# Scores: six of 24 chunks as products of parts, squares in PSUM, norms per partition

## The reference

```python
qn = q / (np.linalg.norm(q, axis=1, keepdims=True) + 1e-06)
kn = k / (np.linalg.norm(k, axis=1, keepdims=True) + 1e-06)
s = kn.transpose(0, 2, 1) @ qn / tau
s = s - s.max(-1, keepdims=True)
a = np.exp(s)
a /= a.sum(-1, keepdims=True) + 1e-09
return (v @ a)
```

## Time and profile before

| | |
|---|---|
| median of 3 runs | 999.54 us (999.44 to 999.87) |
| profiled execution | 1000.11 us, its span 998.3 us |
| PE busy | 992.4 us, 99% |
| DVE, ACT, POOL busy | 852.2, 763.8, 60.4 us |
| granted TensorE clock | 1.00 |
| chain that ended last | PE 97%, DMA 1% |

### The profile page before, as it was taken

One profiled execution on the slowest core, in us unless ns is written; L12 is line 12 of the kernel. 1 busy time (PEld: TensorE's weight loads), 2 busy tenths in 40 slices (PEclk: granted clock), 3 DMA queues, 4 the chain that ended last, 5 costly groups with the idle time before them and its releaser, 6 DMA issues.

```text
span 998.3 us, 14814 instructions
## 1 busy us (share of the span) xinstructions
PE 992.4 (99%) x5355; PEld 899.4 (90%) x5355; DVE 852.2 (85%) x1051; ACT 763.8 (77%) x1181; POOL 60.4 (6%) x55
## 2 busy tenths in 40 slices
PE   9999999999999999999999999999999999999998
PEld 8888989999999999999999888888888888888997
DVE  7779989999999999999896777887888888888886
ACT  6689888999999989999886676666666666666664
POOL 0200001101001011010110000000000000000000
PEclk9999999999999999999999999999999999999999
DMA  9913233635527436353445632543534434434333
GB/s 348 377 23 74 43 59 43 123 95 79 113 40 133 110 51 123 91 78 102 76 52 179 154 112 74 153 105 122 151 79 151 116 95 139 140 95 132 112 98 92
DMA packets 154116, 113.15 MB, mean 113 GB/s; under 512 B 114880, under 2 KB 137536, under 8 KB 154048
## 3 DMA queue, kind: packets, MB, share of 16 engines
q1 hardware_dynamic: 140704, 96.26, 32.6%
q0 software_dynamic: 12736, 15.50, 11.8%
q10 hardware_dynamic: 608, 0.49, 0.2%
HBM read 77.07 MB, written 35.16 MB: 112 GB/s over the span
## 4 chain that ended last, share of the span: by engine, by line
PE 97%; DMA 1%; issue 0%; SPq 0%; DVE 0%; ACT 0%; POOL 0%; DVEq 0%; POOLq 0%
PE banks L1371 50%; PE banks L1572 21%; PE banks L1510 15%; PE banks L1484 7%; PE banks L1381 2%; DMA early_w_in<-w_in 1%; PE banks L1607 0%; PE banks L1399 0%; PE banks L1481 0%; PE banks L1615 0%; SPq L521 0%; SPq L524 0%; ACT early_w_in_parts L427 0%; PE banks L1414 0%; DVE out_tile L1361 0%
## 5 line engine op out<-in xcount | busy, mean ns | idle before, releaser
L1371 PE MATMUL banks<-x_parts,w_in_parts 128*128 128x512 f32 (+1 forms) x1152 | 274.9, 375 | 0.0
L1371 PE MATMUL banks<-xT_parts,a_w_in 128*128 128x512 f32 (+1 forms) x1152 | 259.4, 375 | 0.1
L1371 PEld LDWEIGHTS banks<-x_parts,w_in_parts 128*128 128x128 f32 x1152 | 215.6, 189 | 28.4 <-issue 0.7
L1572 PE MATMUL banks<-g_pair_parts,w_forms 128*128 128x512 f32 (+1 forms) x987 | 239.3, 375 | 0.0
L1371 PEld LDWEIGHTS banks<-xT_parts,a_w_in 128*128 128x128 f32 x1152 | 212.8, 189 | 23.5 <-issue 0.5
L914 ACT ACTIVATE g_pair<-banks 128x512 f32<-128x512 f32 (+1 forms) x192 | 113.0, 588 | 125.2 <-PE banks L1371 118.2
L1572 PEld LDWEIGHTS banks<-g_pair_parts,w_forms 128*128 128x128 f32 x987 | 186.5, 189 | 22.1
L1258 DVE TENSOR_TENSOR g_pair_parts<-g_forms,g_pair_parts 128x1024 fp32r<-128x1024 f32 (+1 forms) x96 | 115.2, 1201 | 23.3 <-ACT g_pair_parts L923 23.1
L1083 DVE SCALAR_TENSOR_TENSOR g_raw<-g_raw,banks 128x1024 f32<-128x1024 f32 (+1 forms) x96 | 114.9, 1197 | 21.0 <-ACT g_raw L792 20.3
L923 ACT ACTIVATE g_pair_parts<-g_forms 128x1024 fp32r<-128x1024 f32 (+1 forms) x96 | 99.4, 1036 | 33.9 <-PE banks L1572 33.3
L792 ACT ACTIVATE g_raw<-g_raw 128x512 f32<-128x512 f32 (+1 forms) x192 | 119.5, 622 | 5.9
(11 more groups left out here) (117 smaller groups left out, 981.8 us busy)
## 6 DMA issues: line engine op xcount, KB each, us to landing
w_forms<-w_forms SPq DMA_DIRECT2D x48, 896.0 KB, 4.7
w_forms<-w_out_forms SPq DMA_DIRECT2D x8, 896.0 KB, 4.2
early_qk<-q SPq DMA_DIRECT2D x23, 256.0 KB, 7.4
early_qk<-k SPq DMA_DIRECT2D x22, 256.0 KB, 7.8
y_raw<-y_parts SPq DMA_DIRECT2D x10, 512.0 KB, 5.4
x_parts<-y_raw SPq DMA_DIRECT2D x40, 128.0 KB, 4.8
out<-out_tile SPq DMA_DIRECT2D x40, 128.0 KB, 2.7
v_in<-v SPq DMA_DIRECT2D x36, 128.0 KB, 4.1
```

What stands on the lines that cost most here:

```text
L1371: mm = pe.matmul(dst, lhsT, rhs, start=first and n == 0, stop=last and n == len(todo) - 1)
L1572: mm = pe.matmul(m_banks[m][:, 0:u.n], ring[k % N_RING][:, form, x, :], by_turns(gp2[k % 2][:, y, operand, 0:u.n]), start=k == 0 and part ...
```

## The change

Six chunks (2, 5, 8, 11, 14, 17) are turned into parts by GpSimd (a copy to `float32r`, then a subtraction) and multiplied by `product`, 12 products in place of 4. Four buffers `early_qk_parts` hold them. PE takes the split chunks in pairs and later than the others: 0, 1, 3, 4, 6, 7, then 2 and 5, and so on. A chunk load into the buffer of a split chunk waits for the split instead of the product. All chunk products read Q from two halves in turn, so the score columns lie in another order, which DVE turns back as it scales them.

ACT writes the squares to PSUM, three pairs of banks (`NSQ` = 3), and DVE adds from there. The sum of one row of the sums to the other is gone: the norm products (`norm_sums`) add both rows in PSUM. These give all sums of q and k with one value to a partition, four columns in bank 2, eight products of one column. One root, one reciprocal of four columns. To have the norms of q along a row again, DVE multiplies the identity by them (two diagonals of 128x128), PE multiplies these by ones (`rq_rows`, bank 7), and DVE copies the result to SBUF. The norm products stand one chunk later than before, `rq_rows` behind the first chunk of head 1. GpSimd starts on w_in1 without waiting for the norms; ACT's roundings of pieces 1 to 3 stand further back.

The second piece of w_in1 moved behind the table load, the third behind the first transposed block, the fourth behind the second exponential. The diff, cut to its core:

```diff
-NQ, NSQ = 14, 4
+NQ, NSQ = 14, 3
+SPLIT = (2, 5, 8, 11, 14, 17)
+N_PARTS = 4
...
+        squares = lambda c: two_banks[1 + c % NSQ][:, :, 0:CHUNKS[c] * C].rearrange("p x (r c) -> p x r c", c=C)
+        turn_of = lambda c: SPLIT[SPLIT.index(c) // 2 * 2 + 1] + 2.5 if c in SPLIT else c
+        IN_BOTH = sorted(range(BOTH), key=turn_of)
+        multiplied = lambda c: IN_BOTH.index(c) + 1
+        def free_parts(eng, c):
+            n = SPLIT.index(c)
+            if n >= N_PARTS:
+                eng.wait_ge(c_mm, multiplied(SPLIT[n - N_PARTS]))
+        part_chunk = lambda c, part: qk_parts[SPLIT.index(c) % N_PARTS][:, part, :, 0:CHUNKS[c], :]
...
-                    sp.wait_ge(c_mm, c - NQ + 1)
+                    if c - NQ in SPLIT:
+                        sp.wait_ge(c_lo, SPLIT.index(c - NQ) + 1)
+                    else:
+                        sp.wait_ge(c_mm, multiplied(c - NQ))
...
-            pool.wait_ge(x_dve, at_dve["q_eps"])
+            for n, c in enumerate(SPLIT):
+                for x in (Q, K):
+                    pool.wait_ge(d_qk[c % NQ][x], qk_loaded(c))
+                free_parts(pool, c)
+                pool.tensor_copy(part_chunk(c, 0), raw_chunk(c)).then_inc(c_hi, 1)
+                pool.wait_ge(c_hi, n + 1)
+                pool.tensor_tensor(part_chunk(c, 1), raw_chunk(c), part_chunk(c, 0).bitcast(F32), ALU.subtract).then_inc(c_lo, 1)
...
-                rows = CHUNKS[c]
-                act.activation(sq[:, c % NSQ, :, 0:rows, :], qk[c % NQ][:, :, 0:rows, :],
-                               ACT.Square).then_inc(c_sq, 1)
+                act.activation(squares(c), raw_chunk(c), ACT.Square).then_inc(c_sq, 1)
...
-            weights_hi(act, IN1, 2)
-            act.wait_ge(x_pe, at_pe["q_sum"])
-            act.activation(rq[:, :], q_ps[:, 0:C], ACT.Sqrt).then_inc(x_act, 1)
-            act.wait_ge(x_pe, at_pe["k_sum"])
-            act.activation(col(K_NORM, CB), k_ps[:, 0:CB], ACT.Sqrt).then_inc(x_act, 1)
+            weights_hi(act, IN1)
+            act.wait_ge(x_pe, at_pe["norm_sums"])
+            act.activation(col(Q_NORM, 2 * CB), norm_ps[:, 0:2 * CB], ACT.Sqrt).then_inc(x_act, 1)
-            weights_hi(act, IN1 + 2, 2)
+            weights_hi(act, IN1 + 1)
...
+            weights_hi(act, IN1 + 2)
+            weights_hi(act, IN1 + 3)
...
-                    dve.tensor_tensor(s, s, sq[:, c % NSQ, :, 0:CHUNKS[c], :], ALU.add).then_inc(c_acc, 1)
-                dve.wait_ge(c_acc, NCH + 1)
-                dve.tensor_tensor(sq_sum[:, :, 0, :], sq_sum[:, :, 0, :], sq_sum[:, :, 1, :], ALU.add).then_inc(c_acc, 1)
+                    dve.tensor_tensor(s, squares(c), s, ALU.add).then_inc(c_acc, 1)
...
-            step("q_eps", lambda: dve.tensor_scalar(rq[:, :], rq[:, :], EPS_NORM, None, ALU.add),
-                 (x_act, at_act["q_norm"]))
-            step("rq", lambda: dve.reciprocal(rq[:, :], rq[:, :]))
+            step("q_eps", lambda: dve.tensor_scalar(col(Q_NORM, CB), col(Q_NORM, CB), EPS_NORM, None, ALU.add),
+                 (x_act, at_act["norms"]))
+            step("k_tau", lambda: dve.tensor_scalar(col(K_NORM, CB), col(K_NORM, CB), EPS_NORM, col(MINUS_TAU),
+                                                    ALU.add, ALU.mult), after="minus_tau")
+            step("rq_rk", lambda: dve.reciprocal(col(RQ, 2 * CB), col(Q_NORM, 2 * CB)))
-                step(f"k_tau{i}", lambda: dve.tensor_scalar(col(K_NORM + i), col(K_NORM + i), EPS_NORM, col(MINUS_TAU),
-                                                            ALU.add, ALU.mult),
-                     (x_act, at_act["k_norm"]), after="minus_tau")
-                step(f"rk{i}", lambda: dve.reciprocal(col(RK + i), col(K_NORM + i)))
+                step(f"diag{i}", lambda: dve.tensor_scalar(diagonal[:, i, :], ident[:, :], col(RQ + i), None, ALU.mult),
+                     (c_const, 3), after="rq_rk")
+            step("rq", lambda: dve.tensor_copy(rq[:, :], rq_ps[:, 0:C]), (x_pe, at_pe["rq_rows"]), after="rq_rk")
-                    s_sb[:, i, :], s_ps[i][:, 0:C], col(RK + i), rq[:, :], ALU.mult, ALU.mult),
-                    (c_mm, BOTH + i + 1), after="rk1")
+                    in_two(s_sb[:, i, :]), turned_back(s_ps[i][:, 0:C], 2), col(RK + i), in_two(rq[:, :]), ALU.mult, ALU.mult),
+                    (c_mm, BOTH + i + 1), after="rq")
...
+                split = c in SPLIT
-                    for x in (Q, K):
-                        if r == 0:
+                    if r == 0 and split:
+                        pe.wait_ge(c_lo, SPLIT.index(c) + 1)
+                    elif r == 0:
+                        for x in (Q, K):
-                        mm = pe.matmul(s_ps[i][:, 0:C], qk[c % NQ][:, K, r, i * P:(i + 1) * P], qk[c % NQ][:, Q, r, :],
-                                       start=c == 0 and r == 0, stop=c == NCH - 1 and r == CHUNKS[c] - 1)
+                        first = c == 0 and r == 0
+                        last = c == NCH - 1 and r == CHUNKS[c] - 1
+                        if split:
+                            parts = qk_parts[SPLIT.index(c) % N_PARTS]
+                            mm = product(s_ps[i][:, 0:C], [(lambda x: parts[:, x, K, r, i * P:(i + 1) * P],
+                                                            lambda x: by_turns(parts[:, x, Q, r, :]))], first, last)
+                        else:
+                            mm = pe.matmul(s_ps[i][:, 0:C], qk[c % NQ][:, K, r, i * P:(i + 1) * P], by_turns(qk[c % NQ][:, Q, r, :]),
+                                           start=first, stop=last)
+            def norm_sums():
+                pe.wait_ge(c_acc, NCH + 1)
+                for x in (Q, K):
+                    for i in range(CB):
+                        n = 2 * x + i
+                        for r in range(CHUNK):
+                            mm = pe.matmul(norm_ps[:, n:n + 1], sq_sum[:, x, r, i * P:(i + 1) * P], ones[:, 0:1],
+                                           start=r == 0, stop=r == CHUNK - 1)
+                mm.then_inc(x_pe, 1)
+            def rq_rows():
+                    pe.wait_ge(x_dve, at_dve[f"diag{i}"])
+                    mm = pe.matmul(rq_ps[:, i * P:(i + 1) * P], ones[:, :], diagonal[:, i, :], start=True, stop=True)
-            for c in range(BOTH):
+            for c in IN_BOTH:
-                if c == BOTH:
-                    q_sum()
-                    k_sum()
+                if c == BOTH + 1:
+                    norm_sums()
...
+                if c == BOTH:
+                    rq_rows()
...
+                if n == 3:
+                    pe.wait_ge(x_dve, at_dve["rq"])

```

29 lines of the change are left out of this document (14 added, 15 removed).

## The result

| | before | after |
|---|---|---|
| median, timed side by side, 6 runs of each | 999.89 us (999.44 to 1000.16) | 1007.03 us (1006.86 to 1007.27) |
| ratio, 95% interval | | 1.0072 (1.0059 to 1.0085) |
| profiled execution, its span | 1000.11, 998.3 us | 1007.27, 1005.5 us |

What follows compares the result with a forecast made beforehand. PE was taken as the bound, with data arrival a floor in the opening. PE's net 0.9 us (2.3 - 1.76 - 0.44 + 0.79) went to data waits; a*w_in1 0.45 earlier took 999.54 to 999.1 us, range 997.7 to 1001.0.

Steps and rivals of the forecast that it cites:

- The step that failed: Plain chunk products: reading Q from two halves in turn costs 0, at most 1.4 us either way over 140 records.
- the waits at chunks 3 and 6: Opening on PE: reordered chunks make it wait for data, 0.6 us at chunk 3 and 0.35 at chunk 6.
- The second term: Norm chain ahead of the score: DVE's copy of the rows takes 0.6 us, drain included, with the score at 44.78.
- the forecast gain of 0.45: Start of a*w_in1 moves from 48.36 to 47.91 us, and the whole kernel gains that 0.45 us.
- The place: Whatever the edit gains or loses is the shift of a*w_in1's start, at 48.36 us; nothing behind it is touched.
- The gain of a split chunk: Chunk products on PE: 1.34 us split against 1.73 plain, 0.39 saved each, 2.3 us for six.
- The floor: Last sum of squares ends at 39.45 us, which no faster product moves; rival that it is reached or passed: 0.09.
- The prediction's account of PE's gain: Opening on PE: of 2.3 us, 1.0 goes to DMA waits, 0.86 to a chunk ahead of the norms; 0.8 earlier.
- DVE and GpSimd did not take turns: Rival, sums beside splits in the opening: the engines take turns, 1010 to 1020 us, or 1005 if partly; chance 0.06.
- A sum that is dearer from PSUM: Rival in the opening: squares into PSUM or sums from it 0.3 us dearer, 1002.3 us; chance 0.05.
- The rival of the norm chain behind GpSimd's first subtraction: Chain held until 42.8 us, 0.1 us lost; with a piece-2 wait and dearer row copy, 999.5; chance 0.22.

Runs made afterwards that it cites:

- e3: The changed kernel with plain products and scores straight, GpSimd writing Q's parts as even columns, then odd: 1000.83 us against 999.79, ratio 1.0009.
- e4: The changed kernel with no chunk split and Q read straight everywhere: 1002.03 us against 999.79 for the kernel before, ratio 1.0020.
- e5: e3 with the norm chain, ACT's order and GpSimd's start of the kernel before: 999.53 us against 999.77, ratio 0.9999.
- e10: e5 without DVE's half-size sum, the norm products adding both rows in PSUM: 999.07 us against 1000.14 for the kernel before, ratio 0.9993.
- e7: e3 with squares in four SBUF buffers and two part buffers instead of four: 1018.0 us against 1000.14 for the kernel before, one run.
- e6: The kernel before with its squares in three pairs of PSUM banks instead of four SBUF buffers: 1000.18 us against 999.77, ratio 1.0003.
- e8: The kernel before with Q read in pairs of columns from its two halves in turn: 1001.79 us against 999.77, one run.
- e9: The kernel before with Q read as all even columns, then all odd ones: 1001.44 us against 999.77, one run.
- e11: The kernel before with Q read in turns of single columns 16 bytes apart: 1010.65 us against 1000.14, one run.

## Why the prediction was wrong

**The step that failed** is "at half that pace the order should cost nothing; the ends, 0.01 us a record dearer or cheaper by the spread of these rows, would be 1.4 us over 140 records, and I take 0". The price is 0.057 us a record, 8.0 us over the 140 plain records. The row it rested on the earlier trace rows is of products from parts. Those do like the turn: 24 of them take 2.92 us in turn and 3.06 straight. A plain product of the same columns does not. The argument went from one form of an instruction to another by its speed alone, as if a slower one asked less of how its operand is read, and then took the end of the range from the spread of rows that had never run this order with this operand. No row of before showed a plain product read in this order, so no row bounded its price, and 140 records multiplied whatever it was. No rival held it either: the slower side was given to contention and to PSUM.

How the 7.63 us between 47.91 and 55.54 close. The norm products come 6.40 us late (46.20 against 39.8). The 120 plain records ahead of them take 5.5 us longer than forecast: 6.84 by their price, less most of the waits at chunks 3 and 6 (0.95 forecast, 0.33 seen at chunk 3) and less the quicker steps into parts. The 72 records of parts take 0.7 us longer (2.92 us for 24, where 2.69 were forecast), and the first chunk starts 0.15 later. From there to the score it is 6.10 us against 4.98 forecast: 10 dearer records stand in between, 0.6 us, and 0.5 us is the copy. From the score to a*w_in1 it is 3.24 against 3.13.

**The second term**, the copy of the rows at 0.6 us "drain included", measures 1.16 us: e3 has 0.20 from the next product on PE (44.39) to the copy and 0.96 from 44.59 to 45.55, with 0.42 of copy and 0.53 of idle time, and the row 45.23 of the earlier trace rows did show an idle time of 0.54 at this same instruction, behind a small operation of DVE's own. The norm chain alone costs 1.85 us (e4), and even with Q read straight the forecast gain of 0.45 becomes a loss of 0.3 in the profiled executions (48.67 against 48.36), of 1.0 us by the medians.

**What held.** The place: everything is the shift of a*w_in1's start, and the stretches behind it are the same. The gain of a split chunk: 24 records of parts in 2.87 us in e3 are 1.44 us a chunk against 1.34 forecast and 1.73 plain. Six times 0.29 is 1.7 us; e4 to e3 shows 1.54. The 2.3 of the forecast were too much, a record of parts being 0.120 here and not the 0.112 of the earlier trace rows. The norm products: 16 records in 1.70 us (1.76). GpSimd: the cast takes 1.03 us, the split 3.5 instead of 4.05, in time for each pair, and no piece of w_in1 was waited for. By the Trainium skill ("GPSIMD Engine Reference", the cycle accounting) the copy was an estimated 1.0 us; the trace agrees with its 1.03 us. The floor: e5 waits for the last sums as soon as PE is early enough.

**What came out near by luck.** The first 48 records of e3 take 11.49 us from start to start, 1.12 above 48 x 0.216, where 0.95 were forecast for waits at chunks 3 and 6. But there is no wait at chunk 3, whose first record stands on the pace at 9.34 us; 1.1 us are already there at the 16th record (9.12 us), from the first records; chunk 6 adds 0.2, and the quick step into parts takes as much off. Both waits are plain only in e10, which starts quicker: 0.95 and 0.51 us from one record to the next at 9.59 and 13.41 us, 1.0 us above the pace in all. The prediction's account of PE's gain, in turn, does not close (2.3 less 1.0 and 0.86 is 0.4, not 0.8): the other 0.4 us stand in the opening before, which is that much longer than 164 x 0.216. Its schedule, from which the forecast comes, is not touched by this.

**The rivals.** DVE and GpSimd did not take turns: a sum beside a split takes 1.23 us, as alone. In e7, where both operands of the sum come from SBUF, they do hold each other up, so this rival described a real mechanism that the squares in PSUM avoid. The Trainium skill ("SBUF — State Buffer", who interferes with whom) draws this line between one SBUF operand and two; the two kernels agree with it. A sum that is dearer from PSUM is refuted by e6 (15.86 us for twelve either way), and a square is no dearer there (1.03 us). The rival of the norm chain behind GpSimd's first subtraction stays untested: in e3 that subtraction ends at 39.04 + 2.35 = 41.39 us, ahead of the first small addition at 42.09, and in the changed kernel at 43.22, ahead of 48.28. The kernel before has such additions beside GpSimd's subtractions, of one column (44.04 and 44.28 us), and they take 0.12 and 0.21 us; none of two columns and no diagonal ran beside one. That rival did name a dearer copy of the rows, by 0.2 us where 0.5 came. The floor was reached in e5 only.

**Left open.** Why a float32 product, which the trace shows as two records, pays for the alternation and one from parts gains by it: the runs show that it does, and for which orders, not by what. Whether a jump back or the number of neighbours read together sets the price (e8, e9, e11). Where the 0.53 us ahead of the first score come from: they are there in every kernel but e10, where the score starts at 43.89, 0.11 us after the last reciprocal. Why up to four of the first steps between records are 0.43 us at a granted clock of 1.00, and how much of the spread between executions that is.

## What to carry to other kernels

The pace of an instruction in some order of access holds for that form of instruction alone. Where a change gives an order to another form, or a type to another order, no row bounds it: give it a wide range on the slow side, multiply it by the count of instructions, and measure it alone first, as one line in the kernel before. When data arrives at a fixed pace, work out the floor first: here six cheaper chunks brought 0.6 to 0.8 us to the start of a*w_in1 in the profiled executions (e5, e10) and 0.2 and 1.1 us by the medians, too little to tell from no change, and beside so small a gain an edit that touches 140 other records has to be free. Before a term of a few tenths is called confirmed, look where in the trace it stands: a sum can come out for another reason.
